# Last two experts' output finished beside their matmuls, expert 7 scattered to the output by token, and slots cut as 3 tiles of 128 and one of 64

## What is computed

```python
    logits = x @ w_gate
    noise_scale = np.log1p(np.exp(x @ w_noise))
    noisy_logits = logits + noise_scale * noise
    top2 = np.argpartition(-noisy_logits, 2, axis=1)[:, :2]
    top2_l = np.take_along_axis(noisy_logits, top2, axis=1)
    top2_l = top2_l - top2_l.max(-1, keepdims=True)
    top2_w = np.exp(top2_l)
    top2_w /= top2_w.sum(-1, keepdims=True) + 1e-09
    for e in range(E):
        for k in range(2):
            mask = top2[:, k] == e
            h = np.maximum(x[mask] @ w1[e], 0.0)
            out[mask] += top2_w[mask, k, None] * (h @ w2[e])
```

## Time and profile before

| | |
|---|---|
| median of three executions | 1003.76 us |
| the profiled execution, its own time | 1000.85 us |
| its span, first to last instruction | 999.0 us |
| TensorE busy | 929.7 us (93%), 5547 matmuls |
| VectorE, ScalarE, GpSimd busy | 523.9, 401.2, 88.8 us |
| mean granted TensorE clock, as a share of full | 0.974 |
| moved by DMA | 117.22 MB |

### The profile page before, as it was taken

How to read it: one execution, slowest core, us unless ns; L and a number is a source line. 1 busy time by engine, 2 the same in 40 slices (tenths; PEclk the granted TensorE clock), 3 DMA queues, 4 the chain that set the end, 5 groups by cost and what they waited for, 6 DMA issues and landing times.

```text
span 999.0 us, 15254 instructions
## 1 busy us (share of the span) xinstructions
PE 929.7 (93%) x5547; PEld 821.6 (82%) x5547; DVE 523.9 (52%) x905; ACT 401.2 (40%) x583; POOL 88.8 (9%) x98
## 2 busy tenths in 40 slices
PE   3999999999999999999999992999999999999970
PEld 2999999999999888888888872888888888888850
DVE  4677778778876544445445533443435345343333
ACT  3556566566565422343235230342324333242210
POOL 3010100100100000003000303000000000000504
PEclk9999999999999999999999995999999999999995
DMA  7041231331602423325232523434525254442517
GB/s 204 2 119 44 92 111 39 108 95 39 218 1 66 146 85 126 127 63 188 87 126 89 205 85 123 161 113 146 181 84 161 100 180 131 152 158 85 155 48 252
DMA packets 72674, 117.22 MB, mean 117 GB/s; under 512 B 5953, under 2 KB 36673, under 8 KB 72641
## 3 DMA queue, kind: packets, MB, share of 16 engines
q1 hardware_dynamic: 68800, 104.20, 32.6%
q0 software_dynamic: 3840, 12.59, 3.8%
HBM read 88.20 MB, written 28.57 MB: 117 GB/s over the span
## 4 chain that ended last, share of the span: by engine, by line
PE 88%; issue 4%; POOL 3%; DMA 2%; DVE 1%; ACT 1%; SPq 1%; POOLq 0%; DVEq 0%
PE psum L635 12%; PE psum L706 10%; PE psum L704 10%; PE psum L705 10%; PE psum L693 9%; PE psum L695 9%; PE psum L694 9%; PE psum L625 7%; PE psum L612 4%; PE psum L613 3%; PE psum L588 2%; PE psum L815 1%; POOL acc L518 1%; PE psum L772 1%; PE psum L600 1%
## 5 line engine op out<-in xcount | busy, mean ns | idle before, releaser
L704 PE MATMUL psum<-down_hi,hid_hi 128*112 128x512 f32 (+1 forms) x448 | 176.8, 395 | 0.0
L706 PE MATMUL psum<-down_hi,hid_lo 128*112 128x512 f32 (+1 forms) x448 | 176.1, 393 | 0.0
L705 PE MATMUL psum<-down_lo,hid_hi 128*112 128x512 f32 (+1 forms) x448 | 174.9, 390 | 0.0
L635 PEld LDWEIGHTS psum<-vx,probs_t 128*128 128x128 f32 x1152 | 141.6, 192 | 0.1
L635 PE MATMUL psum<-vx,probs_t 128*128 128x65 f32 x1152 | 139.4, 271 | 0.0
L872 ACT ACTIVATE probs<-psum,neg_max 128x768 f32<-128x768 f32 x96 | 86.5, 901 | 90.6 <-DVE neg_max L1098 90.2
L1337 DVE SCALAR_TENSOR_TENSOR hid_lo<-psum,hid_hi 128x448 fp32r<-128x448 f32 x64 | 39.9, 624 | 157.0 <-ACT hid_hi L1004 157.0
L1004 ACT ACTIVATE hid_hi<-psum 128x448 fp32r<-128x448 f32 x64 | 34.8, 544 | 203.6 <-PE psum L695 203.6
L1098 DVE TENSOR_REDUCE neg_max<-psum 128x1 f32<-128x768 f32 x96 | 91.7, 955 | 16.2 <-PE psum L613 16.2
L706 PEld LDWEIGHTS psum<-down_hi,hid_lo 128*112 128x112 f32 (+1 forms) x448 | 80.5, 180 | 22.4
L705 PEld LDWEIGHTS psum<-down_lo,hid_hi 128*112 128x112 f32 (+1 forms) x448 | 80.9, 181 | 20.5
(11 more groups left out here) (154 smaller groups left out, 1407.9 us busy)
## 6 DMA issues: line engine op xcount, KB each, us to landing
raw<-in_moe_w SPq DMA_DIRECT2D x64, 512.0 KB, 4.3
raw<-in_moe_w_in SPq DMA_DIRECT2D x24, 512.0 KB, 3.5
raw<-in_moe_w_out SPq DMA_DIRECT2D x24, 512.0 KB, 4.7
slot_x<-zeros SPq DMA_DIRECT2D x7, 1024.0 KB, 5.6
slot_rows<-slot_x SPq DMA_DIRECT2D x8, 896.0 KB, 8.2
slot_y<-y_sb SPq DMA_DIRECT2D x8, 896.0 KB, 4.9
raw_q<-in_q SPq DMA_DIRECT2D x32, 192.0 KB, 3.3
raw_k<-in_k SPq DMA_DIRECT2D x32, 192.0 KB, 3.7
```

The lines of the kernel that those rows point to most:

```text
L635: last = mm(psum[:, 6, i * VW:(i + 1) * VW], probs_t[:, i % 2, j // 3, (j % 3) * P:(j % 3 + 1) * P], vx[:, s, j], start=(j == 0), stop=(j ...
L704: mm(dst, hid_hi[:, f % 2, cols], down_hi[:, slot, f % GP], start=(f == 0), stop=False)
L705: mm(dst, hid_hi[:, f % 2, cols], down_lo[:, slot, f % GP], start=False, stop=False)
L706: last = mm(dst, hid_lo[:, f % 2, cols], down_hi[:, slot, f % GP], start=False, stop=(f == pieces - 1))
```

## The change

It has three parts.

**Slots as 3 tiles of 128 and one of 64.** The 448 rows are loaded, turned and stored as 3 tiles of 128 partitions and one of 64 (`FULL` = 3, `REST` = 64). For the tile of 64 the weights of the matmul are 128 columns wide: `hid_hi` has 512 columns in SBUF, the first 448 are the high parts, and VectorE writes the remainders of the last 64 rows into columns 448 to 511. One matmul against `down_hi` and one against `down_lo` then give high x both parts in partitions 0 to 63 of PSUM and remainder x both parts in partitions 64 to 127. So the tile has two matmuls per piece where a tile had three. The two halves are added when they are evicted: ScalarE copies partitions 64 to 127 to `y_sb`, and VectorE adds partitions 0 to 63. VectorE takes the remainder in two instructions (384 and 64 columns) instead of one, and SP's load and store of the slots are two DMAs each.

**Output finished beside experts 6 and 7.** With `slot_got`, a copy of the slot table in which half-0 slots of expert 6 or above and half-1 slots of expert 7 point to a row of zeros, POOL gathers half 0 after six experts and half 1 after seven. VectorE scales and adds the tiles between the pieces of expert 7 (`combine`): 4 scalings after each of the pieces 0, 1, 2, and 3 additions after each of 3 to 6. SP stores the 12 tiles to the output meanwhile.

**Expert 7's rows by token.** A table in DRAM (`slot_m`) holds for each slot the token (less 1536), the two weights and the low slot; POOL writes it with four more scatters per chunk, after the eight of the rows. The rows of expert 7 are never stored to `slot_y`. POOL gathers for each of its slots the low row of the same token; VectorE scales that, and at the end multiplies each PSUM tile by its weight and adds it (`take_end`), in the order rest tile, 0, 1, 2. POOL scatters each tile to the output rows, with a bound that drops empty slots. TensorE's last two `down` pieces are interleaved in `down_end`.

The core of the diff, its parts for further rounds left out:

```diff
-YR = 112
-YT = CAP // YR
+FULL = CAP // P
+REST = CAP - FULL * P
+YT = FULL + 1
...
             def load_slots(r, e):
 
-                sp.dma_start(slot_rows[0:YR], slot_x[bass.ds(e * CAP, CAP)].rearrange("(j p) n -> p j n", p=YR))\
+                sp.dma_start(slot_rows[:, 0:FULL],
+                             slot_x[bass.ds(e * CAP, FULL * P)].rearrange("(j p) n -> p j n", p=P))\
+                    .then_inc(sx_in, DMA)
+                sp.dma_start(slot_rows[0:REST, FULL], slot_x[bass.ds(e * CAP + FULL * P, REST)])\
                     .then_inc(sx_in, DMA)
...
                 pool.wait_ge(scattered_low, (t + 1) * (DMA * TPC))
+                when(meta_ready, t + 1)
+                for j in range(TPC):
+                    pool.indirect_dma_start(
+                        out=slot_m, out_offset=bass.IndirectOffsetOnAxis(ap=slot_now[:, 1, j:j + 1], axis=0),
+                        in_=meta_now[:, j], in_offset=None).then_inc(meta_scattered, DMA)
...
-            pool.wait_ge(y_stored, LEAD + DMA * (E - 1))
+            pool.wait_ge(redirected, 1)
+            pool.wait_ge(y_stored, LEAD + 2 * DMA * (E - 2))
             for t in range(TILES):
-                gather(acc, 0, t, got_low)
-            pool.wait_ge(y_stored, LEAD + DMA * E)
+                gather(acc, slot_got, 0, t, got_low)
+            pool.wait_ge(y_stored, LEAD + 2 * DMA * (E - 1))
             for t in range(TILES):
-                gather(got, 1, t, got_high[t // 3])
+                gather(got, slot_got, 1, t, got_high[t // 3])
+
+            pool.wait_ge(end_ready, 2)
+            pool.wait_ge(sx_turned, DC * E)
+            for j in range(YT):
+                pool.indirect_dma_start(
+                    out=slot_rows[0:rows_of(j), j], out_offset=None, in_=slot_y,
+                    in_offset=bass.IndirectOffsetOnAxis(ap=end_low[0:rows_of(j), j:j + 1], axis=0))\
+                    .then_inc(end_low_in, DMA)
+
+            pool.wait_ge(stored, DMA * TILES)
+            for i, j in enumerate(ORDER):
+                pool.wait_ge(end_out, i + 1)
+                pool.indirect_dma_start(
+                    out=out, out_offset=bass.IndirectOffsetOnAxis(ap=end_row[0:rows_of(j), j:j + 1], axis=0),
+                    in_=y_sb[0:rows_of(j), j], in_offset=None, bounds_check=N - 1, oob_is_err=False)\
+                    .then_inc(finished, DMA)
...
+            def down_end(f, slot, piece, pieces):
+
+                pe.wait_ge(hid_done, piece)
+                for j in ORDER[0:3]:
+                    down_tile(f - 1, slot, True, j, pieces)
+                pe.wait_ge(hid_done, piece + 1)
+                for i, j in enumerate(ORDER):
+                    if i == 2:
+                        down_tile(f - 1, slot, True, ORDER[3], pieces)
+                    last = down_tile(f, slot, True, j, pieces)
...
+            def combine(f):
+
+                if f == 0:
+                    dve.wait_ge(got_low, DMA * TILES)
+                if f < 3:
+                    for t in range(4 * f, 4 * f + 4):
+                        dv.tensor_scalar(acc[:, t], acc[:, t], weight_now[:, 0, t:t + 1], None, ALU.mult)\
+                            .then_inc(acc_ready, 1)
+                elif f < 7:
+                    dve.wait_ge(acc_ready, TILES)
+                    dve.wait_ge(got_high[f - 3], 3 * DMA)
...
+                elif f == 7:
+                    dve.wait_ge(end_low_in, DMA * YT)
+                    for j in range(YT):
+                        rows = rows_of(j)
+                        chain.mark(dv.tensor_scalar(slot_rows[0:rows, j], slot_rows[0:rows, j],
+                                                    end_meta[0:rows, j, W_LOW:W_LOW + 1], None, ALU.mult))
```

More of the change, by code:

```diff
@@ L39 @@
 LEAD = 1
+TOKEN, W_HIGH, SLOT_LOW, W_LOW = range(4)
+META = 4
 def wait_apart(eng, passed, sem, value):
@@ L712, in down, with layer @@
                     last.then_inc(group_used, 1)
-            def layer(pieces, width, rows, tiles, piece0, group0, chunk, moving_hi, moving_lo, turn, after=None,
-                      turned_in=None):
+            def down_end(f, slot, piece, pieces):
[7 more added lines that the diff above has]
+                    last = down_tile(f, slot, True, j, pieces)
+                    if i < TPC - 1:
+                        last.then_inc(y_ready, 1)
+                last.then_inc(group_used, 1)
+            def layer(pieces, width, rest, piece0, group0, chunk, moving_hi, moving_lo, turn, after=None,
+                      turned_in=None, end=False):
                 for f in range(pieces):
@@ L727, in layer @@
                         pe.wait_ge(y_dve, LEAD + 2 * chunk)
+                    if end and f == pieces - 1:
+                        down_end(f, (f // GP) % RING, piece0 + f, pieces)
+                        return
                     if f >= 1:
-                        down(f - 1, ((f - 1) // GP) % RING, rows, tiles, piece0 + f - 1, pieces)
+                        down(f - 1, ((f - 1) // GP) % RING, rest, piece0 + f - 1, pieces)
                     if after:
@@ L732, in layer @@
                 turn(1)
-                down(pieces - 1, ((pieces - 1) // GP) % RING, rows, tiles, piece0 + pieces - 1, pieces)
+                down(pieces - 1, ((pieces - 1) // GP) % RING, rest, piece0 + pieces - 1, pieces)
             def turn_rows(f, to):
@@ L998, in _, with expert_step @@
             route_last(CHUNKS - 1)
[L1000 removed]
+            def expert_step(n, last, kept, end=False):
                 m0 = EXPERT0 + n * EGR
@@ new lines, in take_end @@
+            def take_end(first, group):
+                for i, j in enumerate(ORDER):
+                    if i < YT - 1:
+                        dve.wait_ge(y_ready, first + i + 1)
+                    else:
+                        dve.wait_ge(group_used, group + 1)
+                    rows = rows_of(j)
+                    one = dv.scalar_tensor_tensor(out=y_sb[0:rows, j], in0=psum[0:rows, j],
+                                                  scalar=end_meta[0:rows, j, W_HIGH:W_HIGH + 1],
+                                                  in1=slot_rows[0:rows, j], op0=ALU.mult, op1=ALU.add)
+                    if j < FULL:
+                        one.then_inc(end_out, 1)
+                        continue
+                    one.then_inc(rest_done, 1)
+                    dve.wait_ge(rest_done, 1)
+                    dve.wait_ge(y_half, E)
+                    dv.scalar_tensor_tensor(out=y_sb[0:rows, j], in0=yt[0:rows, 0],
+                                            scalar=end_meta[0:rows, j, W_HIGH:W_HIGH + 1],
+                                            in1=y_sb[0:rows, j], op0=ALU.mult, op1=ALU.add).then_inc(end_out, 1)
@@ L1368, in _ @@
+            experts(0, 0, combine)
+            done_rounds = chain.base + chain.n
             more = dve.value_load(more_rounds[0:1, 0:1], min_val=0, max_val=ROUNDS - 1)
```

260 lines of the change are left out of this document (181 added, 79 removed).

## The result

| | before | changed |
|---|---|---|
| median of four executions | 1003.25 us | 976.76 us |
| lowest and highest | 1002.45 to 1003.89 | 974.82 to 980.6 |
| profiled execution, its span | 1000.85, 999.0 | 980.6, 978.9 |
| TensorE's last matmul ends (start + 0.23) | 967.32 | 967.27 |
| from there to the end of the span | 31.7 | 11.6 |

The changed kernel takes 0.9734 of the time of before, 95% interval 0.9716 to 0.9752. That is 26.5 us less by the medians. The forecast was 960.8 us, 43.0 less. It had the sign right, but 976.8 lies outside its range of 954 to 969: **16.5 us of the expected gain did not come**.

What follows compares the result with a forecast made beforehand. TensorE, busy 93% of the span, was taken to bound the kernel. Matmuls -19.0, tail -24.7, expert 7's start +0.3 and first load +0.4 sum to -43.0, taking 1003.76 to 960.8 us; range 954 to 969.

Steps and rivals of the forecast that it cites:

- Term 1: Experts' down matmuls: one fewer per piece, 64 in all, and closer spacing of 0.2267 us; -19.0 us.
- the other end, 0.2325: Experts' down matmuls: spacing stays at 0.2325 us if it belongs to the stage, not the shape; -14.9 us.
- the rival that kept 0.2325: Experts' down matmuls: spacing unchanged despite wider weights, gain only 14.9 us, time 964.9 us; chance 0.28.
- the loads lie beside the matmuls in both: Down and dense-layer pieces on TensorE: weight loads, 0.17 and 0.19 us, run beside the matmuls in both.
- Term 2: Program's end after TensorE's last matmul: a tail of 7.0 us instead of 31.7; -24.7 us.
- S: Time origin for the tail forecast: the first of the last down matmuls, at 961.74 us in the kernel before.
- the rival that priced it at 12 us more: Final bounded scatters: slower than before, 1008.8 us if each costs 12 us more; chance 0.01.
- Term 3: VectorE at the start of expert 7: four scalings and a longer remainder cost nothing to 1.5 us; +0.3 taken.
- the covers: Experts 6 and 7: early gathers and stores finish before they are needed, gather waits having 2.2 to 4 us to spare.
- +0.4 for the first load: Expert 0's rows come in two loads that TensorE waits for; 6.09 us may grow by one issue of 0.36.
- VectorE and POOL hinder each other: Expert 7: scalings wait for gathers, pieces 1 and 2's remainders 7.6 us late together, time 967.8 us; chance 0.12.

Runs made afterwards that it cites:

- e1: Changed kernel with all tiles turned as 128 rows, the rest tile's upper half zeroed once; 968.24 us, ratio to before 0.9648.
- e2: Changed kernel with each block's transposes reordered, six tiles of 128 rows first, then two of 64; 971.5 us, ratio 0.9681.
- e6: Kernel before with only the cut of the slots into 3 tiles of 128 and one of 64, old end kept; 996.55 us, ratio 0.9938.
- e9: Changed kernel with the rest tile turned as 96 rows, 32 of them zero, instead of 64; 966.86 us, ratio 0.9644.
- e8: Kernel before, nothing edited, one more execution for a second profile; 1004.31 us.
- e3: Changed kernel with expert 7's four tiles stored by SP as whole blocks, to misplaced rows, instead of scattered by GpSimd; 973.26 us, ratio 0.9704.
- e4: Changed kernel with only expert 7's last tile stored by SP, to a scratch table; three scatters stay on GpSimd; 975.22 us, ratio 0.9713.
- e5: Changed kernel with the three added small start instructions moved to the first dense chunk; 978.33 us, ratio 0.9758.
- e7: e1 with e5's edit and tile 0 finished ahead of the rest tile; 968.34 us, ratio 0.9648.

## Why the prediction was wrong

**Term 1, -19.0 us for the matmuls: right in itself, but not the whole of its part of the change.** The count (704) and the spacing (2.51 us for 11, forecast 2.49) came out, and the other end, 0.2325, which would be 2.56, did not. So the rival that kept 0.2325 falls. The Trainium skill (TensorE: Matmul & The Clock Gate, Back-to-back issue gap) gives 215.8 ns at 512 columns by a formula without the weights; the row says 228. The prediction left out that the same section has this formula for a matmul by itself: where each matmul has a load, it says, both set the spacing, and it gives some 131 ns at 512 columns. The row is far from that as well.

**The step that failed is the one that wasn't taken.** The prediction counted the down matmuls and the loads for them, and doesn't mention the 16 transposes per expert: they stand at nothing in its sum, without a reason. Their number stays the same, but the edit changes their shape: from four tiles of 112 rows to three of 128 and one of 64. The diff shows that, and so does "turned ... as 3 tiles of 128 partitions and one of 64" in the description of the change. A block of eight grew from 0.70 to 1.30 us. Two blocks are 1.20 us an expert; the forecast's period of 40.93 and the measured 42.39 differ by 1.46; 8 x 0.02 of the rest lie in the pieces, and 0.1 I can't place. The first turning grew by 1.6 us, at half the granted clock. e1, e2, e6 and e9 show this from four sides: remove the alternation and 8.5 us come back (e1), halve it and 5.3 (e2), use 96 rows instead of 64 and all of it goes (e9), put the cut in alone and the same periods appear (e6).

The prediction said that "the loads lie beside the matmuls in both". For the down matmuls that is so. In a run of transposes the matmuls are as close as the loads (eight of e1 in 0.79 us, 0.1 each, where a load takes 0.15), so the 0.17 us that a load comes late is lost to TensorE too.

The Trainium skill (TensorE: Matmul & The Clock Gate, LDWEIGHTS) has the time of a load depend on the columns alone and not on the height. The mean of a load, 141 ns at 64 rows and 149 at 128, agrees with it; its own figure for 128 columns, 107 ns, is under both, and the 0.17 us of gap ahead of the load is what it doesn't tell. A reader of that page would have put nothing here, as I did.

**Term 2, -24.7 us for the tail: 4.6 too much.** The chain from the last remainder to the multiply-adds held to 0.2 us. The first scatter started at 967.76, which is S+5.5 where S+4.8 was given, 0.9 us after its tile was ready (966.86), and the fourth at 971.68, which is S+9.4 where S+8.6 to S+9.3 was given. The bounded scatter, of which no row of before showed the kind, costs what a gather does, 0.96 to 1.04 us; the rival that priced it at 12 us more had nothing behind it. SP saw all of it down at 974.9, 7.6 us behind TensorE's end: 0.6 of the error. The other 4.0 us are the drain. The prediction took the landing of the last scatter as the program's end. This is the second step that failed. What it left out is that GpSimd is done with its closing drain only some 6 us after its last DMA instruction, and that moving the last work onto GpSimd brings this to the front. The trace of before has a hint of it: the drain ends 6.4 us behind the last gather there, under the additions. But it doesn't give the length, since that drain ends with VectorE's last addition.

**Term 3 and the covers.** The +0.3 for the start of expert 7 was not seen: from the last turning to TensorE's end e6, which has the old end, takes 47.37 us and the changed kernel 47.46. The +0.4 for the first load was: the stretch of the dense layer to the first turning grew by 0.56 us, of which 0.4 is the later start of the load behind the last scatter's landing and 0.11 its length (6.20 against 6.09). The covers held: `got` was first used at 944.17 and no addition waited. Timeline of GpSimd and VectorE in the piece where most collides, in place of the earlier trace rows:

```profile
936.44 1.19 POOL L568 DMA_INDIRECT got<-slot_y,slot_got  x1 [0.30 <-issue]
...
937.33 1.21 DVE L1242 TENSOR_TENSOR up_lo<-raw,up_hi 128x1024 fp32r<-128x1024 f32 x1
...
937.94 2.65 POOL L568 DMA_INDIRECT got<-slot_y,slot_got  x1 [0.30 <-issue]
938.46 1.21 DVE L1244 TENSOR_TENSOR down_lo<-raw,down_hi 128x1024 fp32r<-128x1024 f32 x1
939.60 1.66 DVE L1507 TENSOR_SCALAR acc<-acc,weight_now 128x512 f32<-128x512 f32 x4
```

The rival "VectorE and POOL hinder each other" was right that they do, and wrong about who pays. VectorE's four scalings take 1.66 us, 0.41 each as before. It is one of GpSimd's gathers that takes 2.65 instead of 0.95, the same one in all eight profiles that have the new end; the eleven others take 0.95 to 1.27, also those beside the same kinds of VectorE's work. The twelve gathers take 17.8 us (933.9 to 951.7) instead of some 15, and the slack ahead of the additions takes that up.

**What is not the change's.** The dense layer starts at 318.23 in the first profile of before, but at 321.24 in the second (e8), and at 318.11 in e9, which has the whole of the change. So 3 to 5 us at the start come and go in either kernel. One cause can be seen in the changed kernel's first stage:

```profile
17.46 1.47 POOL L540 TENSOR_TENSOR raw_q<-raw_q,scale_q 128x768 f32<-128x768 f32 x1 [3.81 <-DMA raw_k<-in_k]
17.78 1.36 DVE L1214 TENSOR_TENSOR onehot<-iota_c,first_hit 128x192 bf16<-128x192 f32 x1
```

and in e9, where GpSimd's instruction starts later than VectorE's:

```profile
17.63 0.36 DVE L1216 TENSOR_TENSOR onehot<-iota_c,first_hit 128x192 bf16<-128x192 f32 x1
17.98 1.47 POOL L541 TENSOR_TENSOR raw_q<-raw_q,scale_q 128x768 f32<-128x768 f32 x1 [4.48 <-DMA raw_k<-in_k]
```

If GpSimd's multiply starts first, VectorE's operation takes 1.36 us instead of 0.36 and ends a little after it; which is first depends on when a load lands. The longer operation delays TensorE's next work by about a microsecond (19.19 in the changed kernel, 18.09 in before). But it doesn't settle when the dense layer starts: e6 has 0.36 and starts it at 320.22, e3 has 1.56 and starts it at 319.80.

What orders the starts is when TensorE's matmuls get to full speed. Windows of TensorE in the first profile of before, from and to, length, busy (matmuls), granted clock, DMA share, GB/s:

```profile
28.00:33.00 5.00, 5.00 (x23) 1.00 0.00 0
38.00:43.00 5.00, 5.00 (x43) 1.00 0.00 2
```

and in the changed kernel:

```profile
33.00:38.00 5.00, 5.00 (x24) 1.00 0.02 3
44.00:49.00 5.00, 5.00 (x43) 1.00 0.00 0
```

TensorE is busy in all four, and yet the later window of each pair has 43 matmuls where the earlier has 23 or 24. In the changed kernel its transposes of `probs` stand 0.21 us apart ahead of 43.1 us and 0.11 behind it. The trace's record of the granted clock has its first entry, full speed, at just these times, 33.03 and 43.10 (the column says 1.00 ahead of them too, where it has no entry). By profile, that entry and the start of the dense layer:

| | full speed from | dense layer from |
|---|---|---|
| e9, before | 32.83, 33.03 | 318.11, 318.23 |
| e3 | 34.51 | 319.80 |
| e6 | 37.23 | 320.22 |
| e8, e4, e1, e2, e5, e7 | 38.24 to 39.29 | 321.24 to 321.96 |
| after | 43.10 | 323.46 |

TensorE starts the work of this stage in e6 when it does in before (18.14 and 18.09), gets full speed 4.2 us later, and starts the dense layer 2.0 us later: half of it, which is what half the rate loses. Why full speed comes at such different times, in either kernel, was not tried.

The 1.3 us after the first turning are the granted clock's. TensorE stands still for 16.8 us ahead of the turning (16.2 before), waiting for the slots, and its clock has fallen to half (0.50, 1.2 GHz) by then, as before. Windows of 4 us, columns as above, first of before and then two of the changed kernel:

```profile
620.00:624.00 4.00, 4.00 (x17) 0.56 0.00 2
```

```profile
628.00:632.00 4.00, 4.00 (x12) 0.50 0.22 19
632.00:636.00 4.00, 4.00 (x17) 0.80 0.60 216
```

After the first up matmul (628.6) half speed lasts to 633.6, 5.0 us; before it lasted from 621.3 to 623.5, 2.3 us. The difference of 2.7 us at half speed costs 1.3. In e1, e6 and e9 this stretch takes 34.71, 35.86 and 34.71 us; e6 has the same turning as the changed kernel and only 0.3 of this loss, and e3 to e5, which turn the same way, take 36.27, 35.65 and 35.92. So at most some tenths are put down to the change.

**The sum again, with the terms as measured:** -43.0 as forecast; +11.6 for turning; +4.6 for the tail. That gives -26.8, against -26.5 by the medians. That they come so close is partly luck, since the start alone moves an execution by more.

**What stays open.** Whether the gap depends on the height of the load or on the width of the moving operand, which shrinks with it in a transpose, was not separated by a run: both are 64, 96 or 128 together. The trace speaks for the height. The late load at 665.90 stands behind a transpose of 128 rows that starts at 665.71, and it is late before the first narrow matmul has begun; in e1 the load behind such a transpose starts with it. The way back costs too: the next load of 128 rows starts 0.20 us behind the start of the transpose of 64. Nor was it tried whether 32 rows cost what 64 do, or whether the drain of GpSimd could be issued sooner or avoided. That the drain has a length of its own rests on e3 alone.

**The better version.** e1 and e9 beat both kernels, at 968.2 and 966.9 us. By the terms as measured, e1 should be at 1003.25 - 43.0 + 4.6 for the tail + 8 x 0.43 for what its periods (41.36) still have above 40.93, which is 968.3. That it was 968.24 owes something to luck, as above. e3 shows what a program that ended without GpSimd would get beyond that, but a scatter by token needs GpSimd here.

## What to carry to other kernels

Count what an edit does to the shape of instructions it doesn't mention. In a run of small matmuls, where loads don't hide, tiles of 64 rows among tiles of 128 cost 0.2 to 0.3 us for each excursion; pad them to 96 or 128 with zeros, or at least group them. And before moving the last work of a program onto an engine, read that engine's closing instructions in the profile: on GpSimd some 6 us followed its last DMA instruction here, and they count only once it ends last.

## What the runs showed of the hardware

- Among transposes with 128 rows of weights (each 128 columns wide), a load of 64 rows has a gap of 0.17 us ahead of it that nothing shown ends, and a block of eight takes 1.30 us with two such excursions, 1.01 with one, and 0.79 with none. At 96 rows it is 0.77, and 0.70 with all eight at 112.
- GpSimd's closing drain took 5.68 us although its last DMA instruction had ended 7.6 us before it, and where its last instructions were the scatters it ended 5.9 to 6.0 us behind the end of the last one (after, e1, e2, e4, e5, e7, e9). Beside VectorE's additions it ended 6.4 to 7.1 us behind (before, e6, e8), each time 0.09 us ahead of the end of the last addition.
- A GpSimd multiply of 768 columns that starts first holds up VectorE's operation with two SBUF inputs for its whole length (1.36 to 1.61 us instead of 0.36). The Trainium skill (SBUF — State Buffer, Who interferes with whom) states this: a VectorE instruction with two SBUF inputs and a GpSimd instruction that reads SBUF share a pair of ports, and whichever starts first keeps it for the whole instruction. The rows agree with it.
- Beside VectorE's splits and scalings one gather's issue went from 0.95 to 2.65 us, while VectorE's four scalings took 0.41 each, as alone. Others beside the same kinds took 0.95 to 1.27, so the rows don't show which of VectorE's instructions held it up.
- In the first stage TensorE's matmuls ran at half the later rate until 32.8 to 43.1 us into the program, from one execution to the next, in both kernels; the start of the dense layer moved with it, from 318.1 to 323.5.
